# Products with v of tile 0 moved behind score 6: four groups of products a pair instead of five

## The chip, the cores and the metric

The kernel runs on one core of one Trainium2 chip. The metric is the device time of one execution in microseconds (us). TensorE does the matmuls and its own weight loads, VectorE, ScalarE and GpSimd work beside it, and SyncE issues most DMAs. A tensor in PSUM, where TensorE writes, is read back by VectorE and ScalarE.

## The reference

Attention with rotary embedding over 4 batches x 8 heads, 576 positions, head size 64, then a mixer (a product over tokens and two over channels). The change is in the attention.

```python
q_rot, k_rot = (rotate(q), rotate(k))
scale = 1.0 / np.sqrt(D)
scores = scale * np.matmul(q_rot, k_rot.transpose(0, 1, 3, 2))
scores = scores - np.max(scores, axis=-1, keepdims=True)
attn = np.exp(scores)
attn = attn / (np.sum(attn, axis=-1, keepdims=True) + 1e-09)
return np.matmul(attn, v).astype(np.float32)
...
h = np.maximum(xt @ w_tok1, 0.0) @ w_tok2
u = x + h.transpose(0, 2, 1)
h2 = np.maximum(u @ w_ch1, 0.0) @ w_ch2
return (u + h2).astype(np.float32)
```

## The kernel before

The 32 heads are done as 16 pairs. A pair has 9 tiles of queries: tiles 0 to 3 are 128 queries each of head A, tile 4 holds the 64 queries left over of both heads, tiles 5 to 8 are head B's. For each tile, in fp32:

- `score(p, i)`: queries times all 576 keys, in two halves of 288 keys, 64 rows of the array each (lines 593 and 589). It writes a slot of two PSUM banks. There are two slots, used in turn by tiles 0, 1, 2, 3, the transposes of the next pair's k, tiles 4, 5, 6, the transposes of the next pair's q, tiles 7, 8. So score 5 takes the slot of the transposes of k, and score 6 that of score 4.
- VectorE takes the maximum of a row (`maximum`, line 801), then ScalarE the exponential (`exponent`, line 715), which frees the slot.
- `turn(p, i)`: ten transposes of the probabilities (line 531, half the rows of the array each) into two banks of `rest`, the same two for every tile. `copy_up` on ScalarE (line 724) and `copy_low` on VectorE (line 810) take one bank each to `pt`, a ring of seven buffers. The next turn waits for both copies and for its own tile's exponential (lines 604 to 606).
- `values(p, i)`: 20 matmuls of the turned probabilities with v and a column of ones (line 633), each 128 rows by 64 columns of the array, summed in two more banks of `rest`. VectorE then divides.

All three engines run a list written out by hand, in order; semaphores hold an instruction, and all behind it on its engine, until what it needs is done. VectorE's list in the middle of a pair reads: `copy_low` of tile 0, guard, `copy_low` of tile 1, `copy_k` (the transposed k of the next pair, line 793), `maximum` 4, `copy_low` 2, `maximum` 5 and 6, `copy_low` 3. ScalarE's: `copy_up` 1 and 2, exponential 4, `copy_up` 3, exponentials 5 and 6, `copy_q`, `copy_up` 4, and so on. In the last pair there is no next one, so the transposes and copies of k and q fall away. After the attention comes the mixer, which the change doesn't touch.

Of the kernel before, what the change touches and what calls it, by code (L numbers as in the profile page):

```python
# [227 lines left out]
def attention(nc, ctx, whole, sb, slot, rest, ident, stage_or_x, raw_qk, rope_sb, rope_half, prob_a, token, wt1, wt2, w1, x_stored,  # L228
# [73 lines left out]
    def no(p):  # L302

        return not 0 <= p < N

    def score_slot(p, i):

        return slot[TURN[p, i] % 2]

    def pt_of(p, i):  # L310

        return pt[(p * TILES + i) % TURNED]
# [7 lines left out]
    def output(h):  # L320

        t0, t1 = HEADS[h]
        return rest[:, 2 + "AB".index(h), 0:(t1 - t0) * V].rearrange("p (t d) -> p t d", d=V)
# [203 lines left out]
    def tensor(pe):  # L527
# [5 lines left out]
        def slot_free(p, i):  # L533

            n = TURN[p, i] - 2
            if n < 0:
                return
            before, what = USERS[n]
            if what in ("k", "q"):
                pe.wait_ge(t_done[what], before + 1)  # L540
            else:
                pe.wait_ge(exped, before * TILES + what + 1)

        def transposes(n, p):

            if no(p):
                return
            if p == 0:
                to = rest[:, 0:2] if n == "k" else rest[:, 2:4]
            else:  # L550
                to = score_slot(p, n)
                slot_free(p, n)
            pe.wait_ge(rotated, 2 * (2 * p + "kq".index(n)) + 2)
            for t in range(NG):
                x = rot[n][p % 2][:, t].rearrange("p h d -> p (h d)")
                for r in range(2):
                    mm = half_turn(to[:, r, t * D:(t + 1) * D], x[(top, low)[r]], r)
            mm.then_inc(t_ready[n], 1)

        def score(p, i):  # L560

            if no(p):
                return
            s, a, t = score_slot(p, i), int(i > G), i - NG * int(i > G)
            slot_free(p, i)
            if i == 0 and p == 0:
                for n in "kq":
                    pe.wait_ge(t_done[n], 1)
                pe.wait_ge(first_moved, 2)
            elif i == 0:  # L570
                pe.wait_ge(tiles_in[0], p * MOVED)
            elif i == G:
                pe.wait_ge(tiles_in[1], (p + 1) * MOVED)
            queries, keys = (turned_x[n][p % 2] for n in "qk")

            def own(r):
                rows = (top, low)[r]
                return queries[rows], keys[rows, r * HALF:(r + 1) * HALF]

            def other(r):  # L580
                rows = (top, low)[r]
                return moved_x["q"][rows], moved_x["k"][rows, :]

            if i == G:

                quarters = [(h, r, (own if h == r else other)(r)) for h in range(2) for r in range(2)]
                for h, r, (x, w) in quarters:
                    out_rows, cols = (top, low)[h], slice(MAIN + h * TAIL, MAIN + (h + 1) * TAIL)
                    mm = pe.matmul(s[out_rows, r, 0:HALF], x[:, cols], w, start=True, stop=True, skip_group_check=True)  # L589
            else:  # L590
                cols = slice(t * P, (t + 1) * P)
                for r, (x, w) in enumerate((own(0), other(1)) if a == 0 else (other(0), own(1))):
                    mm = pe.matmul(s[:, r, 0:HALF], x[:, cols], w, start=True, stop=True, skip_group_check=True)  # L593
            mm.then_inc(scores, 1)

        def turn(p, i):

            if no(p):
                return
            g = p * TILES + i  # L600
            if g == 0:
                pe.wait_ge(t_done["k"], 1)
            else:
                pe.wait_ge(up_done, g)
                pe.wait_ge(low_done, g)
            pe.wait_ge(exped, g + 1)
            for j in range(NG):
                at = j * P if j < G else S - P
                for r, rows in enumerate((top, low)):
                    mm = half_turn(rest[:, r, j * D:(j + 1) * D], prob[i][rows, at:at + P], r)  # L610
            mm.then_inc(turned, 1)

        def values(p, i):

            if no(p):
                return
            g, a = p * TILES + i, int(i >= G)
            pe.wait_ge(up_done, g + 1)
            pe.wait_ge(low_done, g + 1)
            if g == 0:  # L620
                pe.wait_ge(filled, 6)
                pe.wait_ge(t_done["q"], 1)
            if i == 0:
                pe.wait_ge(v_copied, 2 * p + 1)
            if i == G:
                pe.wait_ge(v_copied, 2 * p + 2)
            if p > 0 and i in (0, G):
                pe.wait_ge(x_done, 2 * (p - 1) + a + 1)
            to = output("AB"[a])[:, i - HEADS["AB"[a]][0], :]
            for j in range(NG):  # L630
                for r, cols in enumerate((top, low)):
                    w = v_sb[r if i == G else a][:, j, :]
                    mm = pe.matmul(to[cols], pt_of(p, i)[:, j, cols], w, start=(j == 0), stop=(j == G), skip_group_check=True)  # L633
            mm.then_inc(o_added, 1)
# [5 lines left out]
        for p in range(N):  # L640
            score(p, 0)
            score(p, 1)
            turn(p - 1, 7)
            values(p - 1, 5)
            values(p - 1, 6)
            turn(p - 1, 8)
            score(p, 2)
            score(p, 3)
            turn(p, 0)
            values(p - 1, 7)  # L650
            values(p - 1, 8)
            turn(p, 1)
            transposes("k", p + 1)
            score(p, 4)
            turn(p, 2)
            values(p, 0)
            score(p, 5)
            turn(p, 3)
            score(p, 6)
            values(p, 1)  # L660
            values(p, 2)
            transposes("q", p + 1)
            turn(p, 4)
            score(p, 7)
            score(p, 8)
            turn(p, 5)
            values(p, 3)
            values(p, 4)
            turn(p, 6)


        first, p = slot[0], N
# [227 lines left out]
    def values_left(pool):  # L900

        pool.wait_ge(o_added, N * TILES)

    return Attention(sync=sync, gpsimd=gpsimd, tensor=tensor, scalar=scalar, vector=vector,
                     last_store=last_store, buffers_left=buffers_left, values_left=values_left, slot_left=slot_left)

# [856 lines left out]
```

## Time and profile before

| | |
|---|---|
| runs | 621.3, 621.48, 623.23 us, median 621.48 |
| profiled execution | 619.15 us, span 617.2 us |
| attention (16 pairs) | until about 272 us of the span |
| TensorE matmul busy | 595.7 us, 97% |
| VectorE / ScalarE / GpSimd busy | 443.9 (72%) / 387.3 (63%) / 274.6 us (44%) |
| granted TensorE clock, mean | 0.998 |

A matmul in fp32 is shown by its start and a modelled end; the next one starts before that end, so it is the starts that tell how fast the array goes. "Busy" therefore doesn't mean that nothing waits. PE stands for TensorE's matmuls, PEld for its weight loads, DVE for VectorE, ACT for ScalarE, POOL for GpSimd.

### The profile page before, as it was taken

The page shows a single profiled execution, that of the slowest core. Times are in us where ns is not written, and L with a number is a line of the kernel's source. Part 1 is how long each engine was busy: PE and PEld are TensorE (multiplying, and loading weights), DVE is VectorE, ACT ScalarE, POOL GpSimd, SP SyncE. Part 2 cuts the span into 40 slices and gives each one's busy share as a digit, 9 for nine tenths or more (in the row PEclk, how much of TensorE's full clock was granted, in tenths as well). Part 3 has the DMA queues.
Part 4 walks back from the last instruction along what each step waited for, and adds up shares of the span by engine and source line. Part 5 has one row for each costly group of instructions (what it writes and reads, how often), then busy time and mean ns, then how long its engine had stood idle before and what let it go on. Part 6 is the DMA issues. An engine that isn't in the chain of part 4 may idle for free.

```text
span 617.2 us, 19511 instructions
## 1 busy us (share of the span) xinstructions
PE 595.7 (97%) x7796; PEld 543.1 (88%) x7796; DVE 443.9 (72%) x844; ACT 387.3 (63%) x725; POOL 274.6 (44%) x240
## 2 busy tenths in 40 slices
PE   2999999999999999989999999999999999999997
PEld 1788788788888888879999999999999999999996
DVE  5588788778888888855568876389735699364895
ACT  2566677776666677753736556775567766567753
POOL 4666677776666663348000016820038600168100
PEclk9999999999999999999999999999999999999999
DMA  4235445455456642270005320000310003200002
GB/s 136 74 95 152 127 110 135 133 136 137 135 137 171 169 127 72 58 235 1 1 1 205 86 77 1 1 2 6 107 51 0 0 0 85 78 0 1 1 2 78
DMA packets 49870, 48.18 MB, mean 78 GB/s; under 512 B 12800, under 2 KB 42048, under 8 KB 49792
## 3 DMA queue, kind: packets, MB, share of 16 engines
q1 hardware_dynamic: 49488, 47.00, 26.8%
q8 instruction: 58, 0.95, 0.6%
q14 instruction: 20, 0.16, 0.1%
q10 hardware_dynamic: 304, 0.07, 0.1%
HBM read 30.24 MB, written 9.44 MB: 64 GB/s over the span
## 4 chain that ended last, share of the span: by engine, by line
PE 93%; DVE 2%; DMA 1%; ACT 1%; issue 0%; DVEq 0%
PE rest L633 15%; PE slot L593 12%; PE rest L531 9%; PE slot L1116 8%; PE slot L1118 8%; PE slot L1117 8%; PE rest L1116 6%; PE rest L1118 6%; PE rest L1117 6%; PE slot L1148 2%; PE slot L531 2%; PE slot L589 2%; PE rest L1148 2%; DMA moved_q<-turned_q 1%; PE rest L224 1%; PE rest L221 1%
## 5 line engine op out<-in xcount | busy, mean ns | idle before, releaser
L801 DVE TENSOR_REDUCE neg_max<-slot 128x1 f32<-128x576 f32 x144 | 106.4, 755 | 21.6 <-PE slot L593 16.8
L1107 POOL TENSOR_TENSOR w_ch_part<-w_ch_sums,w_ch_part 128x512 fp32r<-128x512 f32 x21 | 31.0, 1476 | 180.3 <-ACT w_ch_part L1358 180.3
L1422 ACT ACTIVATE pieces<-h 128x288 fp32r<-128x288 f32 x168 | 73.8, 444 | 49.8 <-PE slot L1118 24.5
L633 PE MATMUL rest<-v,pt 128*64 128x65 f32 x2880 | 102.4, 225 | 0.0
L633 PEld LDWEIGHTS rest<-v,pt 128*64 128x64 f32 x2880 | 91.2, 138 | 10.6 <-ACT pt L724 6.2
L810 DVE COPY pt<-rest 128x320 f32<-128x320 f32 x144 | 70.1, 487 | 33.7 <-PE rest L531 33.2
L724 ACT ACTIVATE pt<-rest 128x320 f32<-128x320 f32 x144 | 62.7, 435 | 49.2 <-PE rest L531 48.2
L593 PE MATMUL slot<-turned_k,turned_q 64*128 64x288 f32 x256 | 86.3, 442 | 4.4 <-DMA moved_q<-turned_q 2.0
L593 PE MATMUL slot<-moved_k,moved_q 64*128 64x288 f32 x256 | 86.6, 443 | 0.0
L1513 DVE TENSOR_TENSOR pieces<-h,pieces 128x288 fp32r<-128x288 f32 x168 | 74.4, 453 | 9.3 <-ACT pieces L1422 8.8
L715 ACT ACTIVATE prob_a<-slot,neg_max 128x576 f32<-128x576 f32 x80 | 59.3, 741 | 17.5 <-DVE neg_max L801 14.4
L715 ACT ACTIVATE prob_b<-slot,neg_max 128x576 f32<-128x576 f32 x64 | 47.5, 742 | 12.9 <-DVE neg_max L801 10.3
L593 PEld LDWEIGHTS slot<-turned_k,turned_q 64*128 64x128 f32 x256 | 41.1, 192 | 10.0 <-ACT prob_a L715 4.4
L500 POOL COPY v<-raw_v 128x320 f32<-128x320 f32 x32 | 14.5, 452 | 78.4 <-PE rest L633 78.4
L531 PEld LDWEIGHTS rest<-ident,prob_a 64*128 64x128 f32 x800 | 35.0, 142 | 14.6 <-ACT pt L724 7.5
L593 PEld LDWEIGHTS slot<-moved_k,moved_q 64*128 64x128 f32 x256 | 41.1, 192 | 7.2 <-ACT turned_q L705 6.0
L1580 DVE TENSOR_TENSOR h<-h 128x288 f32<-128x288 f32 x96 | 42.6, 452 | 3.9 <-ACT h L1321 3.8
L361 POOL TENSOR_TENSOR by_sin<-raw_qk,rope_sb 128x640 f32<-128x640 f32 x29 | 44.9, 1550 | 0.0
L360 POOL TENSOR_TENSOR by_cos<-raw_qk,rope_sb 128x640 f32<-128x640 f32 x29 | 44.8, 1544 | 0.0
L531 PE MATMUL rest<-ident,prob_a 64*128 64x64 f32 x800 | 40.5, 230 | 0.8 <-ACT pt L724 0.8
L1358 ACT ACTIVATE w_ch_part<-w_ch_sums 128x512 fp32r<-128x512 f32 x42 | 26.5, 630 | 13.9 <-PE slot L1118 11.6
L531 PEld LDWEIGHTS rest<-ident,prob_b 64*128 64x128 f32 x640 | 28.1, 139 | 7.8 <-ACT pt L724 1.8
(236 smaller groups left out, 1761.3 us busy)
## 6 DMA issues: line engine op xcount, KB each, us to landing
moved_q<-turned_q SPq DMA_DIRECT2D x31, 160.0 KB, 2.7
raw_qk<-in_q_dram SPq DMA_DIRECT2D x16, 256.0 KB, 2.7
raw_v<-in_v_dram SPq DMA_DIRECT2D x16, 256.0 KB, 2.9
x_scratch<-x_pair SPq DMA_DIRECT2D x16, 256.0 KB, 2.7
stage_or_x<-x_scratch SPq DMA_DIRECT2D x16, 256.0 KB, 4.1
raw_qk<-in_k_dram SPq DMA_DIRECT2D x15, 256.0 KB, 2.9
w_ch_whole<-in_moe_w_ch_dram SPq DMA_DIRECT2D x8, 384.0 KB, 3.5
w_ch_A_whole<-in_moe_w_ch_dram SPq DMA_DIRECT2D x4, 768.0 KB, 7.8
```

The lines of the kernel that those rows point to most:

```text
L531: return pe.matmul(to, x, ident[rows, rows], start=True, stop=True, is_transpose=True, skip_group_check=True)
L593: mm = pe.matmul(s[:, r, 0:HALF], x[:, cols], w, start=True, stop=True, skip_group_check=True)
L633: mm = pe.matmul(to[cols], pt_of(p, i)[:, j, cols], w, start=(j == 0), stop=(j == G), skip_group_check=True)
L715: act.activation(prob[i].rearrange("p (f n) -> p f n", f=2), score_slot(p, i)[:, :, 0:HALF], ACT.Exp, bias=neg_max[p % 2][:, i:i + 1]).the ...
L724: act.activation(pt_of(p, i)[:, :, top], rest[:, 0, 0:NG * D].rearrange("p (j n) -> p j n", j=NG), ACT.Copy).then_inc(up_done, 1)
L801: dve.tensor_reduce(neg_max[p % 2][:, i:i + 1], score_slot(p, i)[:, :, 0:HALF], AX.XY, ALU.max, negate=True).then_inc(maxed, 1)
L810: dve.tensor_copy(pt_of(p, i)[:, :, low], rest[:, 1, 0:NG * D].rearrange("p (j n) -> p j n", j=NG)).then_inc(low_done, 1)
L1116: pe.matmul(ps, lhs[0], rhs[0], start=first, stop=False, skip_group_check=True)
L1117: pe.matmul(ps, lhs[0], rhs[1], start=False, stop=False, skip_group_check=True)
L1118: return pe.matmul(ps, lhs[1], rhs[0], start=False, stop=last, skip_group_check=True)
L1422: act.activation(pieces[:, ring(m), 0, :], source[WEIGHTS[n]][:, ft, :], ACT.Copy).then_inc(piece_hi, 1)
L1513: dve.tensor_tensor(pieces[:, ring(m), 1, :], source[WEIGHTS[n]][:, ft, :], f32(pieces[:, ring(m), 0, :]), ALU.subtract).then_inc(piece_lo, 1)
```

## The change

`values(p, 0)`, which stood between turn 2 and score 5, now stands behind score 6, ahead of `values(p, 1)` and `values(p, 2)`. It is done in every pair. Nothing else is edited.

```diff
@@ -653,10 +653,10 @@
             transposes("k", p + 1)
             score(p, 4)
             turn(p, 2)
-            values(p, 0)
             score(p, 5)
             turn(p, 3)
             score(p, 6)
+            values(p, 0)
             values(p, 1)
             values(p, 2)
             transposes("q", p + 1)
```

On TensorE, in the middle of pair 0 (pair 9, whose rows are shown below, reads the same with other buffers), the list was and is as follows. L531 are turns 2 and 3, L593 scores 5 and 6, L633 the products, by the buffer of `pt` that they read; a line starts with - where it stood before, with + where it stands now.

```order
 L531 MATMUL rest<-ident,prob_a 128x64 x10
+L593 MATMUL slot0<-moved_k,moved_q 128x288
+L593 MATMUL slot0<-turned_k0,turned_q0 128x288
+L531 MATMUL rest<-ident,prob_a 128x64 x10
+L593 MATMUL slot1<-moved_k,moved_q 128x288
+L593 MATMUL slot1<-turned_k0,turned_q0 128x288
 L633 MATMUL rest<-v0,pt0 64x65 x10
-L593 MATMUL slot0<-moved_k,moved_q 128x288
-L593 MATMUL slot0<-turned_k0,turned_q0 128x288
-L531 MATMUL rest<-ident,prob_a 128x64 x10
-L593 MATMUL slot1<-moved_k,moved_q 128x288
-L593 MATMUL slot1<-turned_k0,turned_q0 128x288
```

Scores 5 and 6 with turn 3 between them now follow turn 2 directly, and the products of tile 0 stand ahead of those of tiles 1 and 2, which came right behind score 6 before and still follow the last row here (the row of products stands for 20 matmuls in the trace, which counts both column halves). The lists of the other engines are the same as before.

## Rows read from the trace of the kernel before

**Rows 1.** The page: busy time and share; the chain's shares by engine.
```profile
PE 595.7 (97%) x7796; PEld 543.1 (88%) x7796; DVE 443.9 (72%) x844; ACT 387.3 (63%) x725; POOL 274.6 (44%) x240
...
PE 93%; DVE 2%; DMA 1%; ACT 1%; issue 0%; DVEq 0%
```

**Rows 2.** Windows, one pair: length, busy PE, PEld, DVE, ACT, POOL, clock, DMA.
```profile
163.49:178.97 15.48, 15.48 (x335) 12.76 (x334) 12.47 (x26) 10.53 (x20) 10.29 (x11) 1.00 0.51 138
```

**Rows 3.** Timeline, TensorE's matmuls, pair 9: start, us, line, what, count.
```profile
164.07 0.53 PE L531 MATMUL rest<-ident,prob_a 64*128 64x64 f32 x10
164.53 0.81 PE L633 MATMUL rest<-v,pt 128*64 128x65 f32 x20
165.26 0.51 PE L593 MATMUL slot<-moved_k,moved_q 64*128 64x288 f32 x1
...
165.61 0.40 PE L593 MATMUL slot<-moved_k,moved_q 64*128 64x288 f32 x1
...
165.85 0.47 PE L531 MATMUL rest<-ident,prob_a 64*128 64x64 f32 x10
166.15 0.46 PE L593 MATMUL slot<-moved_k,moved_q 64*128 64x288 f32 x1
...
166.79 1.39 PE L633 MATMUL rest<-v,pt 128*64 128x65 f32 x40
168.11 0.53 PE L531 MATMUL slot<-ident,rot_q 64*128 64x64 f32 x10
```

**Rows 4.** Timeline, VectorE, the same stretch; in brackets idle time before.
```profile
163.22 0.49 DVE L810 COPY pt<-rest 128x320 f32<-128x320 f32 x1 [0.28 <-PE rest L531]
163.62 0.81 DVE L793 COPY turned_k<-slot 128x640 f32<-128x640 f32 x1
164.35 0.75 DVE L801 TENSOR_REDUCE neg_max<-slot 128x1 f32<-128x576 f32 x1
165.02 0.48 DVE L810 COPY pt<-rest 128x320 f32<-128x320 f32 x1
166.06 1.60 DVE L801 TENSOR_REDUCE neg_max<-slot 128x1 f32<-128x576 f32 x2 [0.56 <-PE slot L593]
```

**Rows 5.** Timeline, TensorE's weight loads of turn 3, pair 9.
```profile
165.61 0.57 PEld L531 LDWEIGHTS rest<-ident,prob_a 64*128 64x128 f32 x10
```

**Rows 6.** Timeline, TensorE: a turn, then scores with no products between, later.
```profile
175.05 0.53 PE L531 MATMUL rest<-ident,prob_b 64*128 64x64 f32 x10
175.41 0.46 PE L593 MATMUL slot<-turned_k,turned_q 64*128 64x288 f32 x1
...
175.71 0.40 PE L593 MATMUL slot<-turned_k,turned_q 64*128 64x288 f32 x1
```

**Rows 7.** Timeline, ScalarE's copy and the turn that waited for it, after pair 15.
```profile
264.52 0.45 ACT L724 ACTIVATE pt<-rest 128x320 f32<-128x320 f32 x1
...
265.02 0.39 PEld L531 LDWEIGHTS rest<-ident,prob_b 64*128 64x128 f32 x10 [1.00 <-ACT pt L724]
...
265.02 0.53 PE L531 MATMUL rest<-ident,prob_b 64*128 64x64 f32 x10 [0.86 <-ACT pt L724]
```

**Rows 8.** Timeline, ScalarE: the exponential of tile 4, pair 9.
```profile
165.14 0.74 ACT L715 ACTIVATE prob_a<-slot,neg_max 128x576 f32<-128x576 f32 x1
```

**Rows 9.** Pair 0: VectorE's copy, the chain's products of tile 0, turn 3.
```profile
22.20 0.49 DVE L810 COPY pt<-rest 128x320 f32<-128x320 f32 x1
...
22.16 1.28 PE rest L633 x20
...
24.49 0.51 PE L531 MATMUL rest<-ident,prob_a 64*128 64x64 f32 x10
```

**Rows 10.** Pair 15: VectorE's copy, ScalarE's exponential of tile 4, the chain's products.
```profile
257.18 0.48 DVE L810 COPY pt<-rest 128x320 f32<-128x320 f32 x1
...
257.32 0.73 ACT L715 ACTIVATE prob_a<-slot,neg_max 128x576 f32<-128x576 f32 x1
...
259.22 1.32 PE rest L633 x40
```

**Rows 11.** Timeline, TensorE: score 0 of a pair behind a transfer.
```profile
63.02 0.48 PE L593 MATMUL slot<-turned_k,turned_q 64*128 64x288 f32 x1 [1.28 <-DMA moved_q<-turned_q]
```

## The prediction

> **What bounds the kernel now.** I read the page's busy lines first, then its chain that ended last. TensorE is busy for 97% of the span and makes 93% of that chain; VectorE has 2%, ScalarE 1% [rows 1]. So a microsecond of TensorE work or of TensorE waiting is a microsecond of the kernel, unless something shows otherwise. Then I took one steady pair of heads, from the scores of tile 4 of pair 9 to those of pair 10: 15.48 us, with matmuls in flight throughout, VectorE busy for 12.47 of it [rows 2]. Busy over the whole pair says nothing of one stretch, though, so the stretch that the change touches was read instruction by instruction on three engines. On TensorE [rows 3]: turn 2 (the transposes of tile 2's probabilities) starts at 164.07, the 20 products with v of tile 0 at 164.53, score 5 at 165.26, turn 3 at 165.85, score 6 at 166.15, the 40 products of tiles 1 and 2 at 166.79, and the next pair's transposes at 168.11. The reader should see that nothing there waits visibly: each group starts where the one before lets it.
>
> Now VectorE in the same stretch [rows 4]: the copy of turn 1's lower half 163.22 to 163.71, the copy of turned k 163.62 to 164.43, the maximum of tile 4 at 164.35 to 165.10, the copy of turn 2's lower half 165.02 to 165.50. Four operations without a gap; only afterwards does it stand idle (0.56 us, released by score 5). Turn 3 writes the same two banks that this last copy reads and waits for it (line 605). Its first weight loads are at 165.61 [rows 5], 0.11 us after the copy's end. TensorE isn't seen waiting only because the products of tile 0 and score 5 fill just this time. That is the reading on which the forecast rests: between turn 2 and turn 3 the path on VectorE is as long as the one on TensorE.
>
> **The change, part by part.** No operation is added or removed; 20 matmuls a pair go from before score 5 to behind score 6. The other engines' programs are unchanged.
>
> What it removes on TensorE, if nothing waits. Before, from turn 2 to the end of the products of tiles 1 and 2: 168.11 - 164.07 = 4.04 us. After: turn to score 0.36 (175.05 to 175.41 [rows 6]); score 5 to turn 3 0.54, made of 0.30 (175.41 to 175.71 [rows 6]) and 0.24 (165.61 to 165.85 [rows 3]); turn 3 to score 6 0.30; score 6 to the products 0.64; and 60 products. 40 take 1.32 (166.79 to 168.11) and 20 take 0.73 (164.53 to 165.26), so 20 more cost 0.59 and a group by itself has about 0.14 of its own; 60 take 1.91. The sum is 3.75, a gain of 0.29 us a pair.
>
> What stands against it. Without the products, score 5 could start at 164.07 + 0.36 = 164.43; it must also wait for the copy of turned k, whose slot it takes (164.43 plus a handover of 0.05, below), so 164.48. Turn 3 would then be ready at 164.48 + 0.54 = 165.02. But the copy of turn 2's lower half can't come sooner: it stands behind the maximum of tile 4, that behind the copy of turned k, that behind the copy of turn 1's half, and all four are released by TensorE work ahead of turn 2 or by turn 2 itself, none of which moves. It still ends at 165.50. So TensorE stands with an empty array for about 0.5 us, and what filled that time is done later, in the open.
>
> Start of turn 3 after the change. The copy's end plus a handover. Where the array was empty and a turn waited for a ScalarE copy, the copy ended at 264.52 + 0.45 = 264.97 and the loads started at 265.02, 0.05 later [rows 7]. With three semaphores behind each other, and the 0.11 seen before, I take 0.10: 165.60. On an empty array the first matmul starts with its load, as at 265.02, so 165.60 stands against 165.85 before: 0.25 us come back. Then turn to score 0.36: score 6 at 165.96. Score 6 takes the slot of tile 4 and needs its exponential, which ends at 165.14 + 0.74 = 165.88 [rows 8]; with 0.05, 165.93, so it is just not late. Products at 165.96 + 0.64 = 166.60, 60 of them until 168.51. Before it was 168.11. **The cost is 0.40 us a pair.**
>
> Bounds of this term. Below: handover 0.05 and a turn to score of 0.30, where score 6 is then held to 165.93 by the exponential: 166.57 + 1.91 = 168.48, or 0.37. Above: the empty array gives nothing back (the first matmul comes 0.24 behind the loads as before, at 165.85), and the whole 0.59 is added. I take 0.40, since rows 7 show such a start directly.
>
> What is behind it. The wait removed from TensorE's line of work doesn't return elsewhere: the transposes of q, the copy of q and every later score of the pair are placed relative to the products' end, so they slide by 0.40 with it. The maximum of tile 5 comes 0.64 earlier (165.42 instead of 166.06), but its exponential is not what the next groups wait for. The products of tile 0 free a buffer that only the copy of tile 7 uses again, in the next pair: covered. GpSimd's copies of v wait for products 4 and 8, which slide along.
>
> How many pairs. Pairs 1 to 14 repeat the pattern: 14 x 0.40 = 5.6. Pair 0 runs this stretch slowly (its 20 products take 1.28 us instead of 0.73), so the array was at 1.2 GHz; the copy of turn 2 ends at 22.20 + 0.49 = 22.69, when score 5 would still be running (it ends its place at 24.49 now) [rows 9]. No wait there: turn 3 comes about 1.3 us earlier, but score 6 and more then runs at half pace; I take 0, with 1 us to either side. Pair 15 has no copy of k, so VectorE is done sooner relative to turn 2: its copy ends at 257.18 + 0.48 = 257.66; turn 3 at 257.76, score 6 at 258.12 (its exponential ends at 257.32 + 0.73 = 258.05, plus 0.05 is 258.10), products at 258.76 until 260.67. The chain has the products from 259.22 for 1.32, which in starts (0.07 less, as 166.86 in the chain is 166.79 in the rows) is 259.15 to 260.52 [rows 10]. So +0.15.
>
> Sum: 5.6 + 0 + 0.15 = 5.75 us on the profiled execution's 619.15: 624.9. The median of the runs is 621.48, 2.3 us above that execution, so the forecast in that measure is 621.48 + 5.75 = **627.2 us**.
>
> A rule that speaks against this comes from the Trainium skill, TensorEngine Tiling (Array Packing), Key Properties: changing the tiling mode, not only the tile, drains TensorE. The turns and scores use half rows and the products half columns, so one group fewer is two changes of mode fewer. The trace agrees that a change has a price (turn to products 0.46 against turn to score 0.36, and 0.14 behind the products). By that rule alone the sum is rival 1.
>
> **Rivals.**
> 1. *The group's own cost goes and nothing waits.* Then 16 x 0.29 = 4.6 us are saved: 616.8. For it: the costs of a group are in the rows, and no wait on VectorE is named there. It would need turn 3 to be free to start at about 165.02. It decides from the point where the copy of turn 2 ends before that, 0.5 us sooner than it does. Against it: four operations back to back on VectorE, none moved. It could be true only if VectorE's operations ran shorter without the products beside them. Chance 0.08.
> 2. *The wait is there but is paid back.* VectorE and ScalarE are ahead by 0.64 us at tile 5, and small waits later in the pair go. It would have to give back all but 0.1 us of the 0.40: within 0.3% of 621.5. Against it: later groups wait for results of TensorE's own slid work. Chance 0.05.
> 3. *The full 0.59 is added*, because the restart of an empty array costs what it saves: 14 x 0.59 + 0.15, 8.4 us, 629.9. For it: turn 3's loads stand at 165.61 already and can't come much sooner. Against it: rows 7. Chance 0.15.
> 4. *Transfers shift.* Score 0 of one pair waited 1.28 us for the moved q [rows 11]. Its issue and its user both slide, so the wait should stay; a microsecond either way belongs to the range, not to another outcome.
>
> **How the numbers follow.** The forecast has 0.72, rivals 1, 2, 3 have 0.08, 0.05, 0.15. The bounds of a pair (0.37 to 0.59) give 626.8 to 630; a microsecond for pair 0 and one for transfers widen that to 624.6 to 630.2, which leaves out rival 1 and the outer ends. 0.3% is 1.9 us, about what a measurement of this kernel can tell from no change. Slower 0.87, same 0.05, faster 0.08.
>
> **What would show it.** In the profile after, VectorE's four operations stand back to back as before with the same ends relative to turn 2; turn 3's loads and first matmul start together 1.5 us after turn 2 (164.07 to 165.60), with about 0.5 us without a matmul start before them, put down to the copy; 60 products take 1.9 us; pairs take 15.9 us instead of 15.5. I am wrong if turn 3 starts about 1.0 us after turn 2 (rival 1), if the 60 products take clearly less than 1.9 us, or if the pair's period stays though turn 3 waits (rival 2).

## The result, and the profile after

| | before | after |
|---|---|---|
| median of 7 runs | 621.06 us (618.29 to 623.23) | 625.31 us (624.28 to 626.48) |
| ratio | 1 | 1.0072, 95% interval 1.0054 to 1.009 |
| span of the profiled execution | 617.2 us | 624.5 us |
| TensorE / VectorE / ScalarE busy | 595.7 / 443.9 / 387.3 us | 597.0 / 442.6 / 385.5 us |

The change makes the kernel 0.7% slower: the two medians are 4.25 us apart, and the ratio of the runs makes it 4.5 us (3.4 to 5.6). The forecast was slower by 5.75, at 627.2 with a range of 624.6 to 630.2. The profiled executions are not the median ones: before it took 619.15 us, 1.9 below the median of its runs, after it 626.48, the longest of the seven. So the spans differ by 7.3 us, more than the medians do.

The busy lines of the page after answer to [rows 1]. The columns are the same.

```profile
PE 597.0 (96%) x7796; PEld 541.2 (87%) x7796; DVE 442.6 (71%) x844; ACT 385.5 (62%) x725; POOL 274.0 (44%) x240
```

Only TensorE's busy time grew, by 1.3 us, and the ends of its matmuls are modelled; the span grew by 7.3. So most of the growth is waiting. TensorE's matmuls in pair 9, as in [rows 3]:

```profile
166.15 0.53 PE L531 MATMUL rest<-ident,prob_a 64*128 64x64 f32 x10
166.57 0.51 PE L593 MATMUL slot<-moved_k,moved_q 64*128 64x288 f32 x1
...
166.92 0.40 PE L593 MATMUL slot<-turned_k,turned_q 64*128 64x288 f32 x1
167.68 0.53 PE L531 MATMUL rest<-ident,prob_a 64*128 64x64 f32 x10 [0.35 <-issue]
168.01 0.51 PE L593 MATMUL slot<-moved_k,moved_q 64*128 64x288 f32 x1
...
168.70 1.97 PE L633 MATMUL rest<-v,pt 128*64 128x65 f32 x60
170.60 0.53 PE L531 MATMUL slot<-ident,rot_q 64*128 64x64 f32 x10
```

Turn 2 to turn 3 is 167.68 - 166.15 = 1.53 us (before 1.78), turn 2 to the end of the products 170.60 - 166.15 = 4.45 (before 4.04). The last start of score 5 is 0.76 us ahead of turn 3, where 0.24 would do: an empty array for 0.52 us. VectorE in the same stretch, as in [rows 4]:

```profile
165.29 0.49 DVE L810 COPY pt<-rest 128x320 f32<-128x320 f32 x1 [0.28 <-PE rest L531]
165.70 0.82 DVE L793 COPY turned_k<-slot 128x640 f32<-128x640 f32 x1
166.43 0.75 DVE L801 TENSOR_REDUCE neg_max<-slot 128x1 f32<-128x576 f32 x1
167.09 0.48 DVE L810 COPY pt<-rest 128x320 f32<-128x320 f32 x1
167.49 0.75 DVE L801 TENSOR_REDUCE neg_max<-slot 128x1 f32<-128x576 f32 x1
```

They are the same four operations, back to back, and at the same distances from turn 2; only the maximum of tile 5 moved up to them. The weight loads of turn 3 [rows 5] and ScalarE's exponential of tile 4 [rows 8] are now:

```profile
167.65 0.42 PEld L531 LDWEIGHTS rest<-ident,prob_a 64*128 64x128 f32 x10 [0.78 <-ACT pt L724]
```

```profile
166.71 0.44 ACT L724 ACTIVATE pt<-rest 128x320 f32<-128x320 f32 x1 [0.98 <-PE rest L531]
167.21 0.74 ACT L715 ACTIVATE prob_a<-slot,neg_max 128x576 f32<-128x576 f32 x1
```

The loads start at 167.65, 0.08 us after VectorE's copy ends (167.09 + 0.48 = 167.57). The profile puts the wait down to ScalarE's copy (L724), and the matmul's to "issue". But ScalarE's copy ended at 167.15, 0.5 us before the loads. A turn waits for three semaphores, and VectorE's copy is the one of them that ended last. Experiment 1 shows that it was this one.

### The profile page after: what moved, and what is told of

The parts are those of the page before. It is cut to its first block, busy times and chain, and to the rows that moved or that the text cites. A ratio compares the mean times of both kernels' runs of the same rounds, so it can differ in the third digit from the quotient of the medians.

```text
span 624.5 us, 19511 instructions
## 1 busy us (share of the span) xinstructions
PE 597.0 (96%) x7796; PEld 541.2 (87%) x7796; DVE 442.6 (71%) x844; ACT 385.5 (62%) x725; POOL 274.0 (44%) x240
## 4 chain that ended last, share of the span: by engine, by line
PE 91%; DMA 3%; DVE 2%; ACT 2%; issue 1%; DVEq 0%
PE rest L633 14%; PE slot L593 11%; PE rest L531 8%; PE slot L1116 8%; PE slot L1118 8%; PE slot L1117 8%; PE rest L1116 6%; PE rest L1118 6%; PE rest L1117 6%; DMA moved_q<-turned_q 3%; PE slot L1148 2%; PE slot L531 2%; PE slot L589 2%; PE rest L1148 2%; PE rest L224 1%
## 5 line engine op out<-in xcount | busy, mean ns | idle before, releaser
L633 PE MATMUL rest<-v,pt 128*64 128x65 f32 x2880 | 98.7, 224 | 0.0
L633 PEld LDWEIGHTS rest<-v,pt 128*64 128x64 f32 x2880 | 89.6, 137 | 10.0 <-ACT pt L724 6.5
L593 PE MATMUL slot<-turned_k,turned_q 64*128 64x288 f32 x256 | 87.1, 445 | 4.6 <-DMA moved_q<-turned_q 2.2
L724 ACT ACTIVATE pt<-rest 128x320 f32<-128x320 f32 x144 | 62.6, 435 | 45.7 <-PE rest L531 44.8
L593 PE MATMUL slot<-moved_k,moved_q 64*128 64x288 f32 x256 | 87.9, 448 | 0.0
L531 PEld LDWEIGHTS rest<-ident,prob_a 64*128 64x128 f32 x800 | 34.2, 142 | 24.0 <-ACT pt L724 19.5
L593 PEld LDWEIGHTS slot<-turned_k,turned_q 64*128 64x128 f32 x256 | 41.2, 193 | 10.3 <-issue 4.5
L531 PE MATMUL rest<-ident,prob_a 64*128 64x64 f32 x800 | 41.4, 232 | 6.0 <-issue 5.0
L593 PEld LDWEIGHTS slot<-moved_k,moved_q 64*128 64x128 f32 x256 | 41.1, 193 | 6.6 <-ACT turned_q L705 6.0
L531 PEld LDWEIGHTS rest<-ident,prob_b 64*128 64x128 f32 x640 | 28.0, 139 | 7.9 <-ACT pt L724 2.0
```

The lines of the kernel that those rows point to most:

```text
L531: return pe.matmul(to, x, ident[rows, rows], start=True, stop=True, is_transpose=True, skip_group_check=True)
L724: act.activation(pt_of(p, i)[:, :, top], rest[:, 0, 0:NG * D].rearrange("p (j n) -> p j n", j=NG), ACT.Copy).then_inc(up_done, 1)
```

## Experiments

In what follows "the stretch" is the time from the start of turn 2 to the end of the products behind score 6, the median of pairs 1 to 14. Two more sums were taken from each trace. "Waits at score 0" are the times from a pair's turn 6 to the first score of the next pair, less the 0.36 us that a turn takes in front of a score [rows 6], added up. "Periods" are the 14 times from score 4 to score 4 of pairs 1 to 15, less those waits. The periods belong to the order of the work: in the four kernels below with the old order and no added work on VectorE (before, b2, d1, d2) they are 214.8 to 215.2. The waits turned out to vary by themselves.

| kernel | median, us | ratio to before (95%) | turn 3 | score 6 | stretch | periods | waits at score 0 |
|---|---|---|---|---|---|---|---|
| before | 621.06 | 1 | 1.78 | 2.09 | 4.04 | 214.8 | 3.5 |
| after | 625.31 | 1.0072 (1.0054 to 1.009) | 1.54 | 1.87 | 4.455 | 220.9 | 3.9 |
| a1 after, short maximum | 622.87 | 1.0041 (1.0023 to 1.0058) | 1.16 | 1.69 | 4.28 | 218.7 | 3.8 |
| a2 after, both cuts | 620.42 | 1.0004 (0.9979 to 1.0029) | 1.16 | 1.50 | 4.06 | 215.4 | 3.2 |
| b2 before, both cuts | 620.34 | 0.9997 (0.9977 to 1.0018) | 1.78 | 2.09 | 4.04 | 214.9 | 5.1 |
| b1 before, maximum twice | 630.56 | 1.0169 (1.0149 to 1.019) | 2.20 | 2.53 | 4.53 | 221.5 | 7.9 |
| c1 products behind score 5 | 624.81 | 1.0098 (1.0081 to 1.0114) | 1.85 | 2.21 | 4.16 | 216.5 | 7.2 |
| c2 products with tiles 7, 8 | 628.52 | 1.0148 (1.0131 to 1.0165) | 1.54 | 1.87 | 3.87, without the 20 | 221.8 | 6.6 |
| c3 after, k on ScalarE | 622.20 | 1.0054 (1.0041 to 1.0068) | 1.39 | 1.72 | 4.31 | 218.8 | 1.9 |
| c4 after, copy first | 636.08 | 1.0283 (1.0263 to 1.0303) | 1.16 | 2.55 | 5.14 | 230.3 | 1.7 |

Turn 3 and score 6 are counted from turn 2. The kernel before had medians of 620.19 beside a1, a2, b1, b2, and 619.30 beside the c kernels; each ratio is against the runs of the same chip, so rows are compared by their ratios and not by their medians. The c kernels ran 4 to 6 times each.

**1. Shorten VectorE's chain (a1_short_max).**

```diff
-            dve.tensor_reduce(neg_max[...], score_slot(p, i)[:, :, 0:HALF], AX.XY, ALU.max,
+            dve.tensor_reduce(neg_max[...], score_slot(p, i)[:, 0:1, 0:36] if i == G and p > 0 else ..., AX.XY, ALU.max,
```

> The changed kernel, with the maximum of tile 4 taken over 36 of its 576 columns in pairs 1 to 15 (the other 540 are left out), so that VectorE is done with it some 0.6 us sooner. Theory: two waits stand behind the cost of 0.41 us a pair. The first, turn 3 for VectorE's copy of turn 2, shrinks: turn 3 starts about 1.16 us after turn 2 instead of 1.53. The second, score 6 for the exponential of tile 4 (which stands behind ScalarE's copy of turn 2), does not move: score 6 stays about 1.86 us after turn 2, and the 60 products end 4.42 us after turn 2 (4.455 in the changed kernel, 4.04 before). Time 625 us, no gain over the changed kernel. Rival A, that only VectorE's chain holds the stretch: 4.07 us, time 620. Rival B, that the cost lies in the 60 products or the restart itself and in no wait on VectorE: turn 3 stays at 1.53.

Measured: VectorE and TensorE of this kernel, pair 9.

```profile
165.47 0.18 DVE L801 TENSOR_REDUCE neg_max<-slot 128x1 f32<-128x36 f32 x1
165.75 0.49 DVE L810 COPY pt<-rest 128x320 f32<-128x320 f32 x1
```

```profile
165.18 0.53 PE L531 MATMUL rest<-ident,prob_a 64*128 64x64 f32 x10
...
166.34 0.53 PE L531 MATMUL rest<-ident,prob_a 64*128 64x64 f32 x10
166.87 0.51 PE L593 MATMUL slot<-moved_k,moved_q 64*128 64x288 f32 x1
...
167.55 1.97 PE L633 MATMUL rest<-v,pt 128*64 128x65 f32 x60
169.46 0.53 PE L531 MATMUL slot<-ident,rot_q 64*128 64x64 f32 x10
```

Nothing but VectorE's maximum was touched, and turn 3 came 0.37 us sooner (1.16 behind turn 2). The loss to the kernel before is 0.4% instead of 0.7%. So turn 3 had waited for VectorE, and rival B falls. Rival A falls too: score 6 stands 0.53 behind turn 3 instead of 0.33, held by a second wait, and the stretch is 4.28, not 4.07. It is not 4.42 either, and the time fell where none of it was expected to. The exponential came earlier than I had it: ready beforehand, it starts 0.10 us before the copy ahead of it ends (166.08 against 165.74 + 0.44), where in the changed kernel it came 0.06 after.

**2. Cut the second wait as well (a2_short_both), and the control (b2_short_both).**

```diff
-            act.activation(prob[i].rearrange(...), score_slot(p, i)[:, :, 0:HALF], ACT.Exp,
+            f = slice(0, 1 if i == G and p > 0 else 2)
+            act.activation(prob[i].rearrange(...)[:, f], score_slot(p, i)[:, f, 0:HALF], ACT.Exp,
```

> As the kernel before in this list (changed kernel, short maximum of tile 4), and ScalarE's exponential of tile 4 over one of its two halves only (288 of 576 columns, the rest left out) in pairs 1 to 15. Theory: with both waits cut, turn 3 about 1.16 us and score 6 about 1.55 us after turn 2, the products' end at 4.14 us; 0.3 us a pair are gone of the 0.41, time 621 us. Rival B (the 60 products or the restart): stays at 4.4 and 625 us.

> The kernel before the change with the same two cuts (maximum of tile 4 over 36 columns, its exponential over 288, in pairs 1 to 15; the rest of both left out). Theory: the products of tile 0 cover both waits, so nothing is gained: products' end 4.04 us after turn 2, time 621 us, within 1. If the kernel before had hidden waits there, it would gain as the changed one does, up to 4 us.

Measured: with both waits cut the changed order is level with the old one (620.42 against 620.34; stretch 4.06 against 4.04), and the same cuts gain nothing in the old order. Both kernels leave out most of tile 4's maximum and half of its exponential, so they tell of waits and are no orders to use. This is the clean pair: 4.455 to 4.06 in the one, 4.04 to 4.04 in the other. Of the 0.415 us a pair, 0.395 went with these two cuts, and in the old order the 20 products hid both waits.

**3. Lengthen the chain in the old order (b1_double_max).**

```diff
             copy_k(p + 1)
+            if 0 < p < N - 1:
+                dve.wait_ge(scores, p * TILES + 5)
+                ...
+                dve.tensor_reduce(spare_last[:, 0:1], score_slot(p, 4)[:, :, 0:HALF], AX.XY, ALU.max, ...
             maximum(p, 4)
```

> The kernel before the change with the maximum of tile 4 taken twice (once into an unused column) in pairs 1 to 14: VectorE's chain between turn 1 and turn 3 is 0.67 us longer. Theory: the chain was just as long as TensorE's work, to within 0.1 us, so nearly all of it shows: turn 3's first matmul 0.4 us later (2.2 us after turn 2 instead of 1.78), score 6 0.4 to 0.45 later by the exponential, the products' end 4.5 us after turn 2, time 621 + 14 x 0.45 = 627.5 us. Rival: VectorE had slack in this stretch (0.5 us or more): under 1 us in all, 621 to 622.

Measured, VectorE and TensorE in pair 9 (lines are one higher in this kernel, and L865 is the added maximum):

```profile
171.04 0.75 DVE L865 TENSOR_REDUCE spare_last<-slot 128x1 f32<-128x576 f32 x1
171.71 0.75 DVE L802 TENSOR_REDUCE neg_max<-slot 128x1 f32<-128x576 f32 x1
172.37 0.48 DVE L811 COPY pt<-rest 128x320 f32<-128x320 f32 x1
```

```profile
170.76 0.53 PE L532 MATMUL rest<-ident,prob_a 64*128 64x64 f32 x10
171.21 0.80 PE L634 MATMUL rest<-v,pt 128*64 128x65 f32 x20
...
172.95 0.53 PE L532 MATMUL rest<-ident,prob_a 64*128 64x64 f32 x10 [0.25 <-issue]
...
173.97 1.39 PE L634 MATMUL rest<-v,pt 128*64 128x65 f32 x40
175.29 0.28 PE L532 MATMUL slot<-ident,rot_q 64*128 64x64 f32 x2
```

The chain became 0.67 us longer (171.71 - 171.04). The loads of turn 3 start at 172.92, 2.16 us behind turn 2 where they stood at 1.54 before, so 0.62 of the 0.67 shows: the old order had 0.05 us to spare on VectorE. The matmuls of turn 3 moved by 0.42 only, since they now start with their loads. Turn 3 at 2.20 and the stretch of 4.53 are as expected. The time is not: 630.56 instead of 627.5. The spans differ by 11.4 us: 6.7 in the periods, 0.3 in pair 0, and 4.4 in the waits at score 0, which I had not reckoned with. Experiment 7 takes them up.

**4. Where the 20 products stand (c1_behind_score5, c2_with_7_8).**

```diff
 c1:          turn(p, 2)
-            values(p, 0)
             score(p, 5)
+            values(p, 0)
             turn(p, 3)
 c2:          values(p - 1, 8)
+            values(p, 0)
             turn(p, 1)
```

(c2 starts from the changed kernel and has no `values(p, 0)` behind score 6.)

> The kernel before, with the products of tile 0 behind score 5 instead of ahead of it (still five groups, still ahead of turn 3). Theory: what matters is that 20 products lie between turn 2 and turn 3, not where: turn 3 starts 1.80 us after turn 2 (1.78 before), with no wait for the copy; a turn behind products costs 0.36 to the next score instead of 0.30, so the 40 products end at 4.10 us after turn 2 instead of 4.04; time 0 to 1 us above the kernel before. Rival, that the loss of the changed kernel comes from score 5 standing directly behind turn 2: turn 3 waits here too and the time is 3 us or more above.

> Four groups in another way: the products of tile 0 join those of tiles 7 and 8 of the pair before, ahead of turn 1 (from pair 1 on; in pair 0 they stand alone there). Theory: the hole between turns 2 and 3 opens just the same, because VectorE's chain starts with turn 1: turn 3 1.53 us after turn 2, the 40 products end at 3.87 us, and the 0.59 us for the 20 products is paid in the earlier group; together 4.45 a pair, time as the changed kernel, 624 to 626. Rival, that the loss of the changed kernel comes from the 60 products behind score 6 (late release of something behind them): the time is near or under the kernel before, 616 to 621.

Measured, c1 and then c2, pair 9:

```profile
166.16 0.53 PE L531 MATMUL rest<-ident,prob_a 64*128 64x64 f32 x10
...
167.27 0.80 PE L633 MATMUL rest<-v,pt 128*64 128x65 f32 x20
168.00 0.52 PE L531 MATMUL rest<-ident,prob_a 64*128 64x64 f32 x10
168.36 0.46 PE L593 MATMUL slot<-moved_k,moved_q 64*128 64x288 f32 x1
```

```profile
170.23 0.53 PE L531 MATMUL rest<-ident,prob_a 64*128 64x64 f32 x10
...
171.77 0.53 PE L531 MATMUL rest<-ident,prob_a 64*128 64x64 f32 x10 [0.35 <-issue]
...
174.10 0.53 PE L531 MATMUL slot<-ident,rot_q 64*128 64x64 f32 x10
```

In c1 turn 3 follows the products with no wait. Its stretch is 0.12 longer than before (0.06 expected: a score ahead of products takes 0.69, not 0.64), which makes 1.7 us in the periods. Its span is 4.9 us longer: these 1.7 and 3.7 in the waits at score 0, less 0.5 in pair 0. So by its time, 1.0% above the kernel before in four runs, the expectation failed, and by its stretch it nearly held. In c2 the hole between turns 2 and 3 is there again, 1.54 us, though the 60 products now stand in another place: the hole comes from VectorE's chain, not from the large group. Its periods are 7.0 us longer, 0.9 more than those of the changed kernel; its 60 products take 1.98 us to the next turn instead of 1.90. Its time missed the expectation (628.52 instead of 624 to 626); the waits at score 0 in its profile are 6.6 us, 2.7 more than in the changed kernel's.

**5. Take work off the chain (c3_k_on_act).**

```diff
 VectorE:    -            copy_k(p + 1)
              maximum(p, 4)
 ScalarE:     copy_up(p, 1)
             +            copy_next_k(p + 1)
              copy_up(p, 2)
```

> The changed kernel, with the copy of the next pair's transposed k on ScalarE (behind its copy of turn 1, where it stood idle for 1 us) instead of VectorE. Theory: VectorE then starts the maximum of tile 4 when score 4 ends (0.2 us sooner) and its copy of turn 2 0.17 sooner, so turn 3 comes 1.36 us after turn 2 instead of 1.53, score 6 1.70 instead of 1.87, the products' end 4.27 instead of 4.455: 14 x 0.18 = 2.5 us of the loss come back, time about 623. Rival, that the copy of k had no part in it: 625.

Measured: turn 3 at 1.39, stretch 4.31 (expected 1.36 and 4.27), periods 2.1 us below the changed kernel's, 622.20 us. The copy of k had its part in the wait. By its periods it is the fastest order with four groups that leaves nothing out; by its ratio (1.0054 against 1.0072, with intervals that overlap) that isn't certain. It is still slower than five groups.

**6. Turn the order on VectorE (c4_copy_first).**

```diff
-            maximum(p, 4)
             copy_low(p, 2)
+            maximum(p, 4)
```

> The changed kernel, with VectorE's copy of turn 2 ahead of the maximum of tile 4. Theory: turn 3 comes 1.16 us after turn 2 (as with the short maximum), but the maximum is 0.7 us later, and with it the exponential that frees score 6's slot: score 6 only 2.5 us after turn 2, the products' end at 5.1 us: about 10 us slower than the changed kernel, 634. Rival, that only the copy holds this stretch: the products' end at 4.07 us, time 620.

Measured, TensorE in pair 9:

```profile
172.77 0.53 PE L531 MATMUL rest<-ident,prob_a 64*128 64x64 f32 x10
...
173.93 0.52 PE L531 MATMUL rest<-ident,prob_a 64*128 64x64 f32 x10
175.32 0.51 PE L593 MATMUL slot<-moved_k,moved_q 64*128 64x288 f32 x1 [0.87 <-ACT prob_a L715]
```

Turn 3 is early (1.16) and score 6 waits for the exponential (2.55), stretch 5.14, 636.08 us, near the 634 expected. The two results that TensorE needs there both come out of VectorE, and putting one first makes the other late.

**7. The waits at score 0 (d1_before_24, d2_before_104, d3_after_24, d4_c1_24).** Two places of the changed kernel's profile, pairs 11 and 10, one with a long wait and one without. First the chain:

```profile
204.41 3.97 DMA moved_q<-turned_q
208.38 0.14 issue
208.51 1.24 PE slot L593 x8
...
190.54 0.46 PE rest L531 x10
191.00 1.21 PE slot L593 x8
```

Then the queues over the 2 us that start 0.6 us behind the issue of the moved q (packets, MB, share of 16 engines): pair 11, issued at 204.41, and pair 10, issued at 188.13.

```profile
q1 hardware_dynamic: 170, 0.35, 66.4%
q8 instruction: 1, 0.02, 4.4%
...
q1 hardware_dynamic: 173, 0.35, 69.6%
```

The moved q landed after 3.97 us in pair 11 and 2.7 in pair 10. What pair 11 has and pair 10 has not is one packet of 16 KB of instructions, 1.4 us long (4.4% of 16 engines for 2 us). In the traces of all 14 kernels (210 steps from pair to pair), each of the 29 waits of 0.75 us or more has such a packet starting 1.0 to 2.2 us after the issue; 31 steps have one there; the other 179 waited 0.63 at most. The packets of these 29 took 0.9 to 1.8 us, and in each of the 29 the moved q landed 1.1 to 1.4 us after the packet had ended, so the landing followed the packet's end. That is still an association: no experiment switched a packet off. The d kernels were to shift the packets by tiny matmuls at the start:

```diff
         pe.wait_ge(consts, 2)
+        for n in range(24):
+            bank, col = divmod(8 * n, BANK)
+            pe.matmul(slot[0][0:8, bank, col:col + 8], ident[:, 0:8], ident[:, 0:8], start=True, stop=True, ...)
         transposes("k", 0)
```

> The kernel before, with 24 tiny extra matmuls (8 by 8, results unused) on TensorE at its very start, where it idles for rotated k. They only shift where in TensorE's program the 16 KB instruction packets are fetched, by 48 instructions (a packet is fetched about every 5.8 us). Theory: score 0 of a pair waits 0.8 to 1.8 us extra when such a packet runs 1.1 to 1.4 us after the issue of the moved q, beside its packets; in the profile of the kernel before this was so in pairs 2 and 5, and all such waits summed to 3.5 us. Worked out from the trace's instruction counts, 48 instructions more leave no pair hit: sum of waits 1.5 to 2 us, 2 us or more faster than before, about 617.5. Rival, that those waits are chance or come from other transfers: 619 to 620, as before.

> The same with 104 extra matmuls (208 instructions). Theory: 6 to 8 of 14 pairs are hit, the waits at score 0 sum to 8 to 12 us, and the kernel takes 5 us or more longer than before, 624 to 628, with 1 us of that perhaps from the extra matmuls at the start. Rival: within 1 us of before.

> The changed kernel with the 24 tiny matmuls. Theory: its waits at score 0 (3.9 us in its profile) fall to 1.5 to 2 as well, so it takes about 623, and against the kernel before with the same 24 the difference is the change's own cost without the fetches: 14 x 0.41 + 0.2, about 6 us. Rival, that the change's cost is really 4.3 us as the two medians had it: 4.3 between the two padded kernels.

> The kernel with the products of tile 0 behind score 5 (which came out 5.5 us slower than before where 0 to 1 was expected), with the 24 tiny matmuls. Theory: 3.7 to 4 us of that were hits by instruction packets (its waits at score 0 sum to 7.2 us, with hits in pairs 2, 5, 8, 11, 14), so they go: about 619 to 620, some 1.5 us above the kernel before with the same 24. Rival, that the place behind score 5 is costly by itself: 624 stays.

| kernel | median, us | ratio to before (619.77) | periods | waits at score 0 | pairs with 0.75 us or more |
|---|---|---|---|---|---|
| d1 before + 24 | 619.09 | 0.9995 (0.9974 to 1.0016) | 215.2 | 4.4 | 3, 12 |
| d2 before + 104 | 619.62 | 0.9999 (0.9975 to 1.0022) | 215.0 | 4.3 | 1, 4 |
| d3 after + 24 | 624.14 | 1.0067 (1.0047 to 1.0087) | 220.8 | 3.1 | none |
| d4 c1 + 24 | 622.55 | 1.0028 (1.0007 to 1.0048) | 216.4 | 8.9 | 3, 6, 9, 12 |

The extra matmuls as the trace of d1 has them:

```profile
L639 PE MATMUL slot<-ident x48: 169/172/180, 1.5 to 2.7; 128*8 128x8 f32 x48
```

As forecasts of the time, three of the four failed: neither padding of the kernel before moved its median, and c1 came down by 2.3 us, not by 5 (its loss to the kernel before fell from 1.0% to 0.3%). The fall doesn't come with fewer waits in the profile of d4, which is of its longest run: 8.9 us against 7.2. The fourth, d3, came out between its theory (6 us from the change) and its rival (4.3), and settles neither. My shift was also mis-sized: the 24 matmuls stand in the trace as 48, each with its weight load, so the program moved by 96 instructions and not 48. What the profiles do show is that the pairs hit move with the program (2, 5 and then 3, 12 in the kernel before; 2, 5, 8, 11, 14 and then 3, 6, 9, 12 in c1), each with a packet at that moment. That speaks against chance alone, but how often a given kernel is hit from run to run can't be told from one profile of each. What d1 and d3 give for the change is 5.6 us in the periods and 5.05 between the medians.

## Why the prediction was right, point by point

- *VectorE's chain is as long as TensorE's work between turns 2 and 3.* Right, and shown from both sides: longer by one maximum, the old order loses (experiment 3); shorter, the new one gains and the old one doesn't (1 and 2).
- *Turn 3 at 1.53 us behind turn 2, by copy end plus 0.10, first matmul with its load.* Measured 1.53 in pair 9, 1.54 as a median; the handover was 0.08, and the matmul stood 0.03 behind the load.
- *Score 6 at 1.89, just not held by the exponential.* Measured 1.87. The end of the exponential (167.95) and the start of score 6 (168.01) are 0.06 apart, as close as was reckoned, and a1 shows that this second wait holds as soon as the first is gone.
- *60 products in 1.91.* Measured 1.90.
- *0.40 us a pair.* Measured 0.415; the score ahead of the products took 0.69 instead of 0.64, and the turn ahead of the score 0.33 instead of 0.36.
- *Pair 0 nothing, pair 15 0.15.* Measured 0.02 and 0.18. The 0.02 is partly luck. The record of the clock in the traces has it rise from 1.2 to 2.4 GHz in pair 0, and not at the same place: 4.36 us behind score 4 before, 4.91 after, 4.72 in d1, 2.52 in d3. From score 4 of pair 0 to that of pair 1 the four took 17.21, 17.23, 17.36 and 16.34 us. So where the clock rises is worth up to 1 us between these executions, which is what the prediction had allowed.
- *Nothing gives it back later in the pair.* Right: from the end of the products to score 4 of the next pair, less all the time from turn 6 to score 0, it is 10.31 us before and after.
- *Transfers: a microsecond either way.* Too small. In 14 profiles the waits at score 0 summed to between 1.7 and 8.9 us. Between the two profiles here they differ by only 0.4. In these two executions the last products of the attention end 7.15 us later, made of 0.47 at the start of pair 0, 0.02 in it, 6.13 in the periods, 0.36 in these waits and 0.17 at the end. The change's own part, by these sums, is the 6.1 in the periods, of which the stretches make 5.8 (14 times 0.415); the ratio of the runs says 4.5 (3.4 to 5.6), and d1 and d3 say 5.6 and 5.05. Whether the mean wait is smaller in the changed kernel over many runs, or the clock rises sooner, was not measured, so up to 1.6 us stay open.
- *The time, 627.2, and its range.* The median came out at 625.31. Of the 1.9 us between them, 0.4 lie in the starting point (621.48 from three runs, 621.06 from seven) and 1.5 in the change itself, by the medians: the open part above. The bounds of a pair alone gave 626.8 to 630, so the median lies in the range only by the microseconds that were added for pair 0 and for transfers. These make 624.8 to 632; the 630.2 of the range isn't their sum.

The rule on changes of tiling mode (Trainium skill, TensorEngine Tiling (Array Packing), Key Properties) agrees with the price of a group in the rows (0.14 us), though no run takes a change of mode by itself, and it doesn't give the outcome. The prediction's 3.75 us, a saving of 0.29, needs turn 3 at 0.90 us behind turn 2. That sum left out a wait which the prediction names further down: score 5 takes the slot of turned k, whose copy ends at 166.52, and starts at 166.57, 0.42 behind turn 2 and not 0.36, so that turn 3 could come at 0.96 at the earliest. Even in a2, with VectorE's chain shortened, it stood at 1.16: the copy of turn 2 started 0.57 behind the turn's start and took 0.49, as in a1's rows above, so it ended at 1.06. The stretch of a2 was 4.06 against 4.04. So the saving wasn't to be had in this order even without the wait for the maximum.

None of the kernels tried that leave nothing out beats the one before.

## What to carry to other kernels

An instruction group between two others may be the cover for a chain on another engine: before moving it, add up what that engine has to do back to back between the two instructions that meet it, and compare the sum with the starts on the busy engine. Here both were equal within 0.1 us: the trace showed no wait, and the work that was taken out left a hole in its place. The work that moved out cost its full time where it landed, less what the restart gave back.

## What was not expected

- A group that starts on an empty array gave back 0.25 us: turn 3's first matmul stood 0.03 behind its load instead of 0.24, so the loss was 0.41 and not the 0.59 of the 20 products.
- A wait for several semaphores was shown under ScalarE's copy and "issue" (0.78 and 0.35 us), while VectorE's copy was what ended it.
- Packets of instructions run beside the kernel's data, and the profile counts both on the same 16 DMA engines: one of 16 KB comes every 5.8 us or so in the attention, and the moved q, 160 KB, landed after 3.5 to 4.0 us instead of 2.7 in the three places with a long wait of the first two profiles, where one ran beside it. The Trainium skill (Runtime: NRT & Kernel Launch, Instruction fetch mechanics) has the 16 KiB blocks, fetched over a queue of their own, and calls the cost of a boundary mostly hidden; the traces agree with the size, and by the association of experiment 7 the cost here fell on a data transfer on the path.
- An fp32 matmul as written (not a transpose) stands twice in the trace, each time with its weight load: d1's 24 are 48. So a tile's products are 10 matmuls in the program and 20 in the trace, which the text ahead of the prediction put down to the column halves. No duration hangs on it.
